# Two weight slots, not three, converted during attention; key copies one loop sooner; two sums moved between minima

## The reference, cut to what matters

```python
# q, k, v: batch 2, heads 8, tokens 768, dims 64
scores = scale * q @ k.T + bias; scores[~keep] = -1e9
a = exp(scores - max); a = a / (sum(a) + 1e-9); x = a @ v        # -> (2, 768, 512)
u = x + ((x.T @ U) @ V).T
y = u + maximum(u @ w_ch1, 0) @ w_ch2
h = maximum(y @ w_in, 0); hu, hv = split(h)
v_n = (hv - mean(hv)) / sqrt(var(hv) + 1e-6)
out = (hu * (w_spatial @ v_n + b_spatial)) @ w_out
```

## Time and profile before

| | |
|---|---|
| median of 3 runs (lowest to highest) | 524.35 us (523.21 to 524.56) |
| the profiled execution, its time | 524.45 us |
| its span, first to last instruction | 522.6 us |
| TensorE busy | 509.6 us (98%), 2870 matmuls |
| DVE, ACT, GpSimd busy | 197.7, 182.3, 125.6 us |
| mean granted TensorE clock | 0.993 |

### The profile page before, as it was taken

One profiled execution on the slowest core, in us unless ns is written; L12 is line 12 of the kernel. 1 busy time (PEld: TensorE's weight loads), 2 busy tenths in 40 slices (PEclk: granted clock), 3 DMA queues, 4 the chain that ended last, 5 costly groups with the idle time before them and its releaser, 6 DMA issues.

```text
span 522.6 us, 7643 instructions
## 1 busy us (share of the span) xinstructions
PE 509.6 (98%) x2870; PEld 424.7 (81%) x2870; DVE 197.7 (38%) x556; ACT 182.3 (35%) x452; POOL 125.6 (24%) x123
## 2 busy tenths in 40 slices
PE   7999979999999999999999999999999999999997
PEld 6788657787788888888888888888888998888995
DVE  5887648712122513112111321111465246440440
ACT  7888767633222411111010242222443212331121
POOL 6896757234343300000000134232000000000000
PEclk9999979999999999999999999999999999999999
DMA  8814600022222300000000032230000000110002
GB/s 237 284 44 132 231 16 29 2 82 82 80 82 83 119 1 1 0 1 0 0 1 0 2 110 61 90 112 0 1 1 0 1 2 1 61 40 21 1 21 100
DMA packets 12246, 27.88 MB, mean 53 GB/s; under 512 B 2224, under 2 KB 2224, under 8 KB 12208
## 3 DMA queue, kind: packets, MB, share of 16 engines
q1 hardware_dynamic: 10336, 23.96, 14.0%
q10 hardware_dynamic: 1872, 3.41, 1.7%
HBM read 24.22 MB, written 3.15 MB: 52 GB/s over the span
## 4 chain that ended last, share of the span: by engine, by line
PE 85%; POOL 7%; issue 3%; ACT 2%; DMA 2%; DVE 1%; SPq 0%; ACTq 0%; POOLq 0%
PE bank L1034 28%; PE bank L1246 25%; PE bank L1165 25%; POOL qk_split L390 3%; PE bank L1087 2%; DMA qk_raw<-in_qk 2%; PE bank L1054 1%; PE bank L1069 1%; POOL qk_split L388 1%; ACT prob L823 1%; POOL w_slot L437 1%; PE bank L1110 1%; POOL V_stack L422 1%; POOL v_all L410 1%; PE bank L1135 1%
## 5 line engine op out<-in xcount | busy, mean ns | idle before, releaser
L1246 PE MATMUL bank<-hid,w_slot 128*128 128x512 f32 x576 | 139.2, 390 | 0.0
L1165 PE MATMUL bank<-u_split,w_slot 128*128 128x512 f32 x576 | 138.7, 390 | 0.0
L1246 PEld LDWEIGHTS bank<-hid,w_slot 128*128 128x128 f32 x576 | 107.7, 188 | 23.2 <-issue 0.9
L1165 PEld LDWEIGHTS bank<-u_split,w_slot 128*128 128x128 f32 x576 | 107.7, 188 | 22.4 <-issue 0.2
L689 DVE SCALAR_TENSOR_TENSOR hid<-bank,hid 128x512 fp32r<-128x512 f32 x48 | 33.2, 692 | 189.5 <-ACT hid L927 189.3
L927 ACT ACTIVATE hid<-bank 128x512 fp32r<-128x512 f32 x48 | 28.7, 598 | 202.9 <-PE bank L1165 202.9
L823 ACT ACTIVATE prob<-prob,row_min 128x256 f32<-128x256 f32 (+1 forms) x96 | 45.9, 479 | 18.6 <-DVE row_min L527 18.6
L1034 PE MATMUL bank<-sp_slot,vn 128*128 128x384 f32 x288 | 50.3, 334 | 0.0
L1034 PEld LDWEIGHTS bank<-sp_slot,vn 128*128 128x128 f32 x288 | 50.0, 188 | 0.2
L429 POOL TENSOR_TENSOR w_slot<-stage,w_slot 128x1024 fp32r<-128x1024 f32 x13 | 31.2, 2396 | 44.9 <-ACT w_slot L877 44.9
L429 POOL TENSOR_TENSOR in_slot<-stage,in_slot 128x1024 fp32r<-128x1024 f32 x4 | 9.6, 2394 | 127.0 <-ACT in_slot L877 127.0
(11 more groups left out here) (94 smaller groups left out, 484.9 us busy)
## 6 DMA issues: line engine op xcount, KB each, us to landing
stage<-in_w_ch SPq DMA_DIRECT2D x16, 512.0 KB, 3.3
qk_raw<-in_qk SPq DMA_DIRECT2D x23, 256.0 KB, 4.7
v_all<-in_v SPq DMA_DIRECT2D x12, 256.0 KB, 4.9
out_dram<-o_stage ACTq DMA_DIRECT2D x12, 256.0 KB, 2.0
stage<-in_w_spT SPq DMA_DIRECT2D x6, 384.0 KB, 3.0
stage<-in_w_in SPq DMA_DIRECT2D x4, 512.0 KB, 3.2
stage<-in_w_out SPq DMA_DIRECT2D x2, 512.0 KB, 3.5
V_raw<-in_V SPq DMA_DIRECT2D x4, 96.0 KB, 4.7
```

The lines of the kernel that those rows point to most:

```text
L1165: last = mm(h_bank[g % 2][:], w_slot[f][:, a, k * P:(k + 1) * P], u_split[c][:, m, k, :], start=(k == 0 and p == 0), stop=(k == KD - 1 and ...
L1246: last = mm(c_ring[(KD * c + k) % 6][:], w_slot[f][:, a, 512 + k * P:512 + (k + 1) * P], hid[g % 2][:, m, :], start=(f == 0 and a == HI an ...
```

## The change

- `EARLY` becomes 2. SP no longer loads slot 2 inside the attention branch but in the loop that follows it. Its low half, two instructions on GpSimd before, becomes one.
- ACT rounds slot 0 at the end of step 9, as before, and slot 1 at the end of step 19 (before: 11). Slot 2, before at step 15, now follows hidden block 0, and every later slot follows one block later.
- GpSimd takes slot 0's low halves in loops 10 and 13 and slot 1's in loops 20 and 22 (before: loops 11 to 16 for three slots).
- GpSimd copies global keys for quad `g+3` in loop `g` (before: `g+2`). `copy_k` itself is unchanged, so in loop `g` it now waits for the scores of quad `g+1`.
- On DVE the sums by dims of quads 0 and 1 are taken between the two halves of the minima of quads 2 and 3 (before: behind both halves). From quad 2 on nothing moves.

```diff
-    EARLY = 3
+    EARLY = 2
...
-                load_stage(2)
...
-                    if 4 <= g + 2 < QUADS:
-                        copy_k(g + 2)
+                    if 4 <= g + 3 < QUADS:
+                        copy_k(g + 3)
...
-                    if 11 <= g < 17:
-                        split_early((g - 11) // 2, (g - 11) % 2)
+                    if g in (10, 13):
+                        split_early(0, g // 13)
+                    if g in (20, 22):
+                        split_early(1, g // 22)
...
-            def score_bias(g):
+            def score_bias(g, half=None):
...
-                for m in range(2):
+                for m in range(2) if half is None else (half,):
...
-                    if s >= 1:
+                    if s >= 3:
                         take_oT(s - 1)
...
-                    if 0 <= s + 2 < QUADS:
+                    if s in (0, 1):
+
+                        score_bias(s + 2, 0)
+                        take_oT(s)
+                        score_bias(s + 2, 1)
+                    elif 0 <= s + 2 < QUADS:
                         score_bias(s + 2)
...
-                    if s in (9, 11, 15):
-                        split_stage({9: 0, 11: 1, 15: 2}[s])
+                    if s in (9, 19):
+                        split_stage(s // 19)
```

## The result

| | before | after |
|---|---|---|
| median, four runs each on one chip (lowest to highest) | 524.31 us (523.21 to 524.56) | 517.73 us (517.53 to 517.82) |
| the profiled execution, its time | 524.45 us | 517.66 us |
| its span | 522.6 us | 515.9 us |
| first hidden block starts at | 104.62 us | 97.84 us |

The changed kernel is faster: the ratio is 0.9878, with an interval of 0.9861 to 0.9895. Between the profiled executions lie 524.45 - 517.66 = 6.79 us, and the first hidden block starts 104.62 - 97.84 = 6.78 us sooner. So everything was won during attention, and the two networks behind it take as long as before.

A forecast was written before the change was run, and what follows sets the result against it. TensorE, busy for 98% of the span, was taken as the bound, its largest wait 3.1 us for quad 18's key copy. Gains of 3.1 + 2.6 + 0.55 = 6.25 us from 524.45 gave 518.2 us, range 517.0 to 520.9.

The forecast's parts named there:

- Slot 2 leaves attention: GpSimd's key copy of quad 18 no longer stands behind slot 2, so TensorE's whole wait goes: 3.1 us won.
- The slow clock behind the wait: From scores of quad 18 to 19, full clock returns once the wait is gone: 2.6 us won.
- Sums by dims: At attention's start, TensorE's waits of 1.01 and 0.57 us go, but ACT limits the gain: 0.55 us won.
- Slot 0's first half ahead: GpSimd's values copy of quad 11 and value tile 6 come 4.2 us later but still in time: 0.
- Slot 1's rounding in step 19: ACT's 1.04 us rounding before the probabilities does not delay the weighing of quad 20: 0, at most 1.0 us.
- Key copies sooner: GpSimd waits in loop g for scores of quad g+1 without holding TensorE: 0, otherwise once 2.0 us.
- Slot 2 after attention: Behind hidden block 0, slot 2 is ready 1.95 us before hidden block 2 reads it: 0.
- Rival (a): The wait goes, but another short one lowers the clock or it falls at the same place: 520.8 us; chance 0.10.
- Rival (b): Value tile 6 lands late, costing 1.2 us at the weighing of quad 12: 519.4 us; chance 0.08.
- Rival (c): Key copy of quad 18 still late because GpSimd is held elsewhere: 523.5 to 524.4 us; chance 0.04.
- Rival (d): Weights come too late in the first network; 532 us if fourteen slots are each 1 us late; chance 0.03.

The follow-up runs named there:

- the slots alone: Changed kernel with key copies put back to quad g+2 in loop g; two early slots and sums between the minima stay: 517.83 us, ratio 0.987.
- The filled wait: Kernel before, with eleven unused identity matmuls on TensorE just ahead of its wait for quad 18's key copy: 521.84 us, ratio 0.996.
- the sums alone: Kernel before, with only the sums by dims of quads 0 and 1 taken between the minima: 522.64 us, ratio 0.9971.
- The last experiment: Changed kernel with an unused one-column copy added on ACT at the end of step 15: 518.15 us, ratio 0.989.
- the run with one early slot: Changed kernel with EARLY = 1, so only slot 0 is converted in attention and slot 1 after it: 542.61 us, ratio 1.0343.
- the rounding in step 17: Changed kernel with slot 0 rounded in step 17 instead of 9, low halves in loops 18, 20 and 21, 22: 517.26 us; run again 517.46 us.

## Why the prediction was right

The forecast was 518.2 us, and the median is 517.73, within its own range. Point by point:

- *Slot 2 leaves attention* (3.1): the wait of 3.06 us went whole. The copy of quad 18 was put near 62, with some 7 us to spare; it ran at 62.51 and had 7.3. The run with the slots alone shows that this part suffices.
- *The slow clock behind the wait* (2.6): 2.63 in the profiled executions. The filled wait shows that the two belong together. But this term is that of the execution that was profiled. In others the slow stretch costs less (1.4 us in the run with the sums alone, and about half of the times of the kernel before lie some microsecond lower), and 517.73 is 5.6 below a median of 523.37 as well as 6.6 below 524.31. The forecast of the time doesn't suffer, since it says what remains. A gain stated from one profile would have been off by a microsecond.
- *Sums by dims* (0.55): this term was too small, 0.74 to 0.77. The turn of x starts at 17.65, as it was worked out. What I left out is that DVE's next minima are sooner as well. They start at 17.60, before at 18.35, with them ACT's next copy of x is 0.78 sooner. Before, the turn in step 3 starts at 20.90, just behind the end of that copy at 20.80; now the copy ends at 20.01 and the turn starts at 20.19. That the turn waited for the copy is read from these times; the profile names no releaser. I had stopped following at TensorE's list, where the lead was 0.59.
- *Step 22 to 23*: 0.28 that were not in the sum. I had counted no gain for roundings that leave ACT's steps, and bounded it by 1.0. The last experiment puts the 0.28 on what stands in ACT's list ahead of that step, where three roundings stood before, one of them in step 15, and two stand after; how one instruction does it stays open.
- *Slot 0's first half ahead* (0): right. `copy_v` of quad 11 ends at 48.55, 1.5 us before the weighing of quad 11 at 50.03 (worked out: near 49.4, 1.4 to spare), and value tile 6 landed 2.3 us after its issue. With the order undone the time is the same.
- *Slot 1's rounding in step 19* (0): the weighing of quad 20 takes its 1.09 us without a wait. A rounding is not free everywhere, though: the one in step 9, in both kernels, costs 0.37.
- *Key copies sooner* (0): right; without it the time is the same.
- *Slot 2 after attention* (0): 1.95 us to spare were worked out, 1.96 are in the rows.

The two missed amounts, 0.2 and 0.28, have the same sign and make the 0.5 us by which the forecast was high. Rival (a), the clock, is refuted for this place. The sign that I gave, a granted clock of 1.00 throughout attention, holds in the first profile of the changed kernel but not in every execution: the last section shows one in which the clock fell near the start. Rival (b) was a matter of one transfer, which landed in 2.3 us. Rival (c) did not come up. Rival (d) had the right mechanism and the wrong distance: it comes at one slot of lead, not at two. When I foretold the run with one early slot I made the mistake of the sums again, and followed only one engine: I counted the path's length but not how little work lies between a hidden block and the next when the lead is one.

## What to carry to other kernels

A wait on the bounding engine can come from the order of an idle engine's list: GpSimd was busy for a quarter of the time, and yet a weight that nobody needed for 40 us stood ahead of a copy that was needed at once. Either moving the weight or moving the copy ahead cured it, and moving the one that isn't urgent left no second wait. Before a lead of prefetched weights is cut, add up conversion from the moment its trigger is free, and compare it with the work that lies between trigger and use: here two slots leave 2 us, and one slot costs 25.

## What the runs showed of the chip

- A wait of 3.06 us was followed by a stretch at TensorE's lower clock, 0.50 of full, whose place and length differ between executions. In the profile of the kernel before the clock stood at 0.50 from 73.0, while TensorE still waited, to 79.5, and scores of quad 18 to 19 took 6.53 us. With the sums alone it was still 1.00 when TensorE went on at 73.13, stood at 0.50 from 74.5 to 77.0, and the step took 5.32 us. The mean granted clocks of the kernel before go with its times: 0.993 with 524.2 to 524.9, 0.996 and 0.997 with 523.0 to 523.4, and once 0.999 with 521.84, which is as if there were no slow stretch. A wait of 1.29 us in almost the same place left the clock at 1.00. The Trainium skill (TensorE: Matmul & The Clock Gate, Terms) would price the stretch with the sums alone, 6.7 us at 0.75, at 1.7 us, an estimate by its rule. The rows have 5.32 - 3.90 = 1.42, again somewhat less than the rule, as 2.63 was less than 3.1.
- Some executions of most kernels here lie some 2.8 us above the rest (520.65 beside 517.66, for one) with a mean granted clock of 0.99 to 1.00 as usual. One was profiled, in the run with one more instruction on ACT. The loss is at the very start: the first 24 matmuls of the scores took 2.83 us there and 1.56 in the changed kernel, and by quad 2 it was 3 us behind. The record of the granted clock says 1.00 for that stretch, in both. First that run, then the changed kernel:

```profile
6.35 2.83 PE L1062 MATMUL bank<-qk_split 64*128 64x128 f32 x24 [0.18 <-DVE qk_split L511]
```

```profile
6.18 1.56 PE L1060 MATMUL bank<-qk_split 64*128 64x128 f32 x24
```

A third profile, of the changed kernel run again (518.88 us), speaks for the clock as the cause. TensorE waited 1.10 us ahead of the same 24 matmuls, the record shows 0.50 from about 8.1 to 11.4 us, and scores of quad 2 started 1.94 us late; the first hidden block was 1.24 us late:

```profile
6.58 2.22 PE L1060 MATMUL bank<-qk_split 64*128 64x128 f32 x24 [1.10 <-DVE qk_split L511]
8.73 2.50 PE L1032 MATMUL bank<-ident 128*128 128x128 f32 x10
```

The ten turns of the identity took 2.50 us at the recorded 0.50. They took 2.50 in the execution above as well, whose record says 1.00, and 1.38 in the changed kernel's first profile. So that execution very likely ran at the lower clock too, and the record missed it; this is argued from the durations and not shown. A wait of 0.75 us at the same place, when the rounding in step 17 was run again, left the clock at 1.00. What decides between the starts was not tried.
